# An attention batch in plain fp32, with its own order of stages on each engine, ahead of a two-layer feed-forward kernel

## The reference

```python
k_p = k.reshape(B, H, Sp, pool, D).mean(axis=3)          # B = 8, H = 8, S = 576, Sp = 72, pool = 8, D = 64
v_p = v.reshape(B, H, Sp, pool, D).mean(axis=3)
scores = scale * np.matmul(q, k_p.transpose(0, 1, 3, 2))
scores = scores - np.max(scores, axis=-1, keepdims=True)
attn = np.exp(scores)
attn = attn / (np.sum(attn, axis=-1, keepdims=True) + 1e-09)
x = np.matmul(attn, v_p)                                  # then (4608, 512)
h = x @ w_in;   x = np.maximum(0.01 * h, h) @ w_out       # w_in 512x2048, w_out 2048x512
h = x @ w_in2;  x = (h * np.clip(h + 3, 0, 6) / 6) @ w_out2
```

## Time and profile before

| | us |
|---|---|
| median of 3 runs | 1704.76 (1704.0 to 1704.78) |
| the profiled execution's own time | 1704.56 |
| its span, first to last instruction | 1702.8 |
| PE busy | 1675.4, 98% of the span |
| DVE, ACT, POOL busy | 1007.7, 627.9, 395.3 |
| start of the first tile on PE | 44.13 |
| end of the eight parts of its step 0 | 50.97 |

### The profile page before, as it was taken

One profiled execution on the slowest core, in us unless ns is written; L12 is line 12 of the kernel. 1 busy time (PEld: TensorE's weight loads), 2 busy tenths in 40 slices (PEclk: granted clock), 3 DMA queues, 4 the chain that ended last, 5 costly groups with the idle time before them and its releaser, 6 DMA issues. The chain is left out here.

```text
span 1702.8 us, 32933 instructions
## 1 busy us (share of the span) xinstructions
PE 1675.4 (98%) x10460; PEld 1489.4 (87%) x10460; DVE 1007.7 (59%) x1807; ACT 627.9 (37%) x1329; POOL 395.3 (23%) x427
## 2 busy tenths in 40 slices
PE   7999999999999999999999999999999999999999
PEld 6777888888888888888999888988989898989898
DVE  6767777676676867765455555444545454444444
ACT  4544433333333433333323333333333333333333
POOL 6226551021120212112432112121111212121200
PEclk8999999999999999999999999999999999999999
DMA  6745778768686786858787757666756675757562
GB/s 197 244 154 195 260 253 247 234 202 278 197 260 222 227 261 204 273 179 280 234 271 245 251 174 227 175 222 176 223 180 222 174 226 174 227 173 227 173 202 75
DMA packets 215810, 366.83 MB, mean 215 GB/s; under 512 B 22464, under 2 KB 47040, under 8 KB 215744
## 3 DMA queue, kind: packets, MB, share of 16 engines
q1 hardware_dynamic: 215744, 366.04, 68.1%
HBM read 308.28 MB, written 57.67 MB: 215 GB/s over the span
## 5 line engine op out<-in xcount | busy, mean ns | idle before, releaser
L1431 PE MATMUL ps_h<-xs_hi,ring 128*128 128x256 f32 x3808 | 814.8, 283 | 10.6 <-ACT p L1056 4.9
L1431 PEld LDWEIGHTS ps_h<-xs_hi,ring 128*128 128x128 f32 x3808 | 642.8, 189 | 56.4 <-issue 15.9
L1431 PE MATMUL ps_h<-xs_lo,ring 128*128 128x256 f32 x1904 | 534.3, 281 | 0.0
L1431 PEld LDWEIGHTS ps_h<-xs_lo,ring 128*128 128x128 f32 x1904 | 358.1, 188 | 25.7
L939 ACT ACTIVATE g_hi<-gate 128x512 fp32r<-128x512 f32 x288 | 181.9, 632 | 397.7 <-DVE gate L1137 212.7
L1384 PE MATMUL ps_y<-g_hi,wout_hi 128*128 128x512 f32 x576 | 225.7, 392 | 0.4 <-DVE y_stage L1192 0.4
L1386 PE MATMUL ps_y<-g_hi,wout_lo 128*128 128x512 f32 x576 | 225.4, 391 | 0.0
L1385 PE MATMUL ps_y<-g_lo,wout_hi 128*128 128x512 f32 x576 | 225.2, 391 | 0.0
L1196 DVE TENSOR_TENSOR u<-ps_h,p 128x256 f32<-128x256 f32 x272 | 114.3, 420 | 186.8 <-PE ps_h L1431 152.1
L1385 PE MATMUL ps_y<-wout_lo,g_hi 128*128 128x512 f32 x576 | 224.2, 389 | 0.0
L1386 PE MATMUL ps_y<-wout_hi,g_lo 128*128 128x512 f32 x576 | 224.2, 389 | 0.0
(11 more groups left out here) (115 smaller groups left out, 1994.2 us busy)
## 6 DMA issues: line engine op xcount, KB each, us to landing
ring<-w_in_split SPq DMA_DIRECT2D x920, 256.0 KB, 2.8
w_in_split<-ring SPq DMA_DIRECT2D x56, 256.0 KB, 3.5
w_in_split<-stage SPq DMA_DIRECT2D x56, 256.0 KB, 3.6
k_raw<-in_kT SPq DMA_DIRECT2D x32, 288.0 KB, 3.8
q_raw<-in_qT SPq DMA_DIRECT2D x32, 288.0 KB, 5.3
v_raw<-in_v SPq DMA_DIRECT2D x32, 288.0 KB
x0T<-x_stage SPq DMA_DIRECT2D x32, 288.0 KB, 3.8
x1T<-y_stage SPq DMA_DIRECT2D x36, 256.0 KB, 5.0
```

The lines of the kernel that those rows point to most:

```text
L1431: mm = pe.matmul(banks[BANK_OF[r]], a, b[:, r, c, :], start=r in OPENS and c == 0 and n == 0, stop=c == 1 and n == 2, skip_group_check=True)
```

## The change

- The first batch's product with the values is one plain fp32 matmul for each head (`pT_f`, `v_f`) in the place of three fp32r matmuls. DVE's `pT_lo` and POOL's `v_sum` and `v_lo` of that batch are gone.
- The keys of units 2 and 3 are summed by DVE in one instruction each, not by POOL in three.
- `FIRST_STAGES` is replaced by three lists, one for each engine. DVE takes the scores of the next unit ahead of normalizing the one before. ACT's roundings 3 to 7 stand at the end. PE has six of the eight parts of step 0 of the first tile (`upper`, `lower`) behind and between the last stages of unit 3, and so no longer as one block.
- The turned half 1 of unit 3 uses unit 0's buffers (`half_buffers`).
- `keep_warm` stands at other places, with other counts, and writes to whichever bank is idle. Ahead of the first scores there are 8 such matmuls, not 13.

```diff
-FIRST_STAGES = [("sum_k", 0), ("sum_k", 1), ("place_k", 0), ("place_k", 1), ("scores", 0),
...
-                ("round", 7), ("turn_p1", 3), ("split_x", 2), ("pv1", 3), ("split_x", 3)]
+FIRST_DVE = [("sum_k", 0), ("sum_k", 1), ("scores", 0), ("scores", 1), ("sum_k", 2),
+             ("normalize", 0), ("divide", 0), ("scores", 2), ("sum_k", 3), ("normalize", 1),
+             ("divide", 1), ("scores", 3), ("normalize", 2), ("divide", 2), ("normalize", 3),
+             ("divide", 3), ("split_x", 0), ("split_x", 1), ("split_x", 2), ("split_x", 3)]
+FIRST_ACT = [("place_k", 0), ("place_k", 1), ("exp", 0), ("exp", 1), ("place_k", 2),
+             ("turn_p0", 0), ("exp", 2), ("pv0", 0), ("place_k", 3), ("round", 0),
+             ("turn_p1", 0), ("turn_p0", 1), ("pv1", 0), ("exp", 3), ("round", 1), ("pv0", 1),
+             ("turn_p1", 1), ("turn_p0", 2), ("split_x", 0), ("round", 2), ("pv1", 1),
+             ("pv0", 2), ("turn_p1", 2), ("turn_p0", 3), ("split_x", 1), ("pv1", 2),
+             ("turn_p1", 3), ("split_x", 2), ("pv0", 3), ("round", 3), ("pv1", 3),
+             ("split_x", 3), ("round", 4), ("round", 5), ("round", 6), ("round", 7)]
+FIRST_PE = [("scores", 0), ("scores", 1), ("scores", 2), ("turn_p0", 0), ("pv0", 0),
+            ("scores", 3), ("turn_p1", 0), ("pv1", 0), ("turn_p0", 1), ("pv0", 1),
+            ("turn_p1", 1), ("turn_p0", 2), ("pv1", 1), ("pv0", 2), ("turn_p1", 2),
+            ("turn_p0", 3), ("pv1", 2), ("turn_p1", 3), ("upper", 0), ("pv0", 3), ("upper", 1),
+            ("pv1", 3), ("upper", 2), ("lower", 0), ("lower", 1), ("lower", 2), ("upper", 3),
+            ("lower", 3)]
+
 WARM_UP = 8
-WARM_STAGES = {("place_k", 0): 0, ("place_k", 1): 3, ("scores", 0): 5, ("place_k", 2): 4,
-               ("turn_p0", 0): 8, ("pv0", 0): 5}
+WARM_STAGES = {("scores", 1): 4, ("scores", 2): 11, ("pv0", 0): 3, ("scores", 3): 5,
+               ("turn_p1", 0): 1, ("pv1", 0): 3, ("pv0", 1): 3, ("turn_p1", 1): 2,
+               ("pv0", 2): 2, ("turn_p1", 2): 2, ("pv1", 2): 1}
...
+        def half_buffers(b, c, half):
+
+            return units[0] if first(b) and c == PAIRS - 1 and half == 1 else buffers(b, c)
...
                 for hd in range(2):
-                    nc.gpsimd.tensor_tensor(u.v_hi[:, hd, hd * D:(hd + 1) * D],
+                    nc.gpsimd.tensor_tensor(u.v_f[:, hd, hd * D:(hd + 1) * D],
                                             raw_v[:, hd, :, 0], raw_v[:, hd, :, 1], ALU.add
-                                            ).then_inc(v_hi_ready, 1)
-                nc.gpsimd.tensor_tensor(u.v_sum[:], raw_v[:, :, :, 0], raw_v[:, :, :, 1],
-                                        ALU.add).then_inc(v_summed, 1)
-                pool.wait_ge(v_summed, c + 1)
-                v_lo(0, c)
+                                            ).then_inc(v_ready, 1)
+                pool.wait_ge(v_ready, 2 * c + 2)
+                pool.sem_inc(v_summed, 1)
...
-                    nc.scalar.activation(u.pT_hi[:, :, 0:n_q], u.ps[0:KEYS, :, 0:n_q], ACT.Copy
+                    to = at.pT_f if first(b) else at.pT_hi
+                    nc.scalar.activation(to[:, :, 0:n_q], at.ps[0:KEYS, :, 0:n_q], ACT.Copy
                                          ).then_inc(pT_hi_ready, 1)
...
+                    if first(b):
+                        pe.wait_ge(pT_hi_ready, half + 2 * n + 1)
+                        for hd in range(2):
+                            mm = pe.matmul(at.ps[:, half, 0:n_q], u.v_f[:, hd, :],
+                                           at.pT_f[:, hd, 0:n_q], start=hd == 0,
+                                           stop=hd == 1)
...
             def first_step(i):
...
+                if i == 0:
+
+                    for m in range(HF):
+                        place(m)
+                    return
                 first_part(i, 1, 0)
...
+            for name, c in FIRST_PE:
+                if name in ("upper", "lower"):
+                    first_part(0, int(name == "upper"), c)
+                else:
...
+                    keep_warm(WARM_STAGES.get((name, c), 0), idle)
                     stage(name, 0, c)
             for i in range(HF):
                 first_step(i)
```

More of the change, by code:

```diff
@@ L374, in wait_k_sum @@
         def wait_k_sum(eng, b, c):
-            if first(b) and c < 2:
+            if first(b):
                 eng.wait_ge(first_k_summed, c + 1)
@@ L790, in _ @@
             for u in units:
-                pool.memset(u.v_hi[:].bitcast(F32), 0.0).then_inc(v_zeroed, 1)
-                pool.memset(u.v_lo[:].bitcast(F32), 0.0).then_inc(v_zeroed, 1)
-            pool.wait_ge(v_zeroed, 2 * PAIRS)
-            pool.sem_inc(k_summed, 2)
-            sum_k(2, 0)
-            sum_v(0, 2)
-            sum_k(3, 4)
-            sum_v(1, 6)
-            sum_v(2, 8)
-            sum_v(3, 10)
+                pool.memset(u.v_f[:], 0.0).then_inc(v_zeroed, 1)
+            pool.memset(units[0].v_hi[:].bitcast(F32), 0.0).then_inc(v_zeroed, 1)
+            pool.memset(units[0].v_lo[:].bitcast(F32), 0.0).then_inc(v_zeroed, 1)
+            pool.wait_ge(v_zeroed, PAIRS + 2)
+            pool.sem_inc(k_summed, PAIRS)
+            pool.sem_inc(v_hi_ready, 2 * PAIRS)
+            pool.sem_inc(pT_ready, 2 * PAIRS)
+            for c in range(PAIRS):
+                sum_v(c, 2 * c)
             blocks_lo(0)
@@ L1474, in stage @@
                     half = int(name[-1])
+                    at = half_buffers(b, c, half)
                     pe.wait_ge(prob_ready, 2 * n + half + 1)
+                    if at is not u:
+                        pe.wait_ge(x0_copied, 2)
                     for hd in ((0, 1), (1, 0))[half]:
-                        if half == 1 and hd == 0:
+                        if half == 1 and hd == 0 and at is u:
                             pe.wait_ge(x0_copied, 2 * n + 1)
@@ L1488, in stage @@
                     half = int(name[-1])
-                    pe.wait_ge(pT_ready, 2 * n + half + 1)
+                    at = half_buffers(b, c, half)
+                    n_q = PART_QUERIES[half]
                     if half == 0:
                         pe.wait_ge(v_ready, 2 * n + 2)
-                    for hd in range(2):
-                        n_q = PART_QUERIES[half]
-                        mm = product(u.ps[:, half, 0:n_q], (u.v_hi[:, hd, :], u.v_lo[:, hd, :]),
-                                     (u.pT_hi[:, hd, 0:n_q], u.pT_lo[:, hd, 0:n_q]),
-                                     hd == 0, hd == 1)
+                    if first(b):
+                        pe.wait_ge(pT_hi_ready, half + 2 * n + 1)
[4 more added lines that the diff above has]
+                    else:
+                        pe.wait_ge(pT_ready, 2 * n + half + 1)
+                        for hd in range(2):
+                            mm = product(u.ps[:, half, 0:n_q],
+                                         (u.v_hi[:, hd, :], u.v_lo[:, hd, :]),
+                                         (u.pT_hi[:, hd, 0:n_q], u.pT_lo[:, hd, 0:n_q]),
+                                         hd == 0, hd == 1)
                     mm.then_inc(pv_done, 1)
@@ L1574, in _ @@
             pe.wait_ge(zeroed, 2)
-            keep_warm(WARM_UP)
-            pe.wait_ge(v_zeroed, 2 * PAIRS)
+            keep_warm(WARM_UP, ps_y[:, DC - 1])
+            pe.wait_ge(v_zeroed, PAIRS + 2)
             pe.wait_ge(kT_zeroed, PAIRS)
-            for i, (name, c) in enumerate(FIRST_STAGES):
-                if name in ("scores", "turn_p0", "pv0", "turn_p1", "pv1"):
-                    if i < FIRST_STAGES.index(("place_k", PAIRS - 1)):
-                        keep_warm(WARM_STAGES.get((name, c), 2))
+            idle = ps_y[:, DC - 1]
+            for name, c in FIRST_PE:
+                if name in ("upper", "lower"):
+                    first_part(0, int(name == "upper"), c)
+                else:
+                    if (name, c) == ("turn_p1", 0):
+                        pe.wait_ge(shifted, 4)
+                        idle = ps_h[:, 0]
+                    if (name, c) == ("turn_p0", 1):
+                        idle = ps_att[:, 0]
+                    keep_warm(WARM_STAGES.get((name, c), 0), idle)
                     stage(name, 0, c)
```

41 lines of the change are left out of this document (13 added, 28 removed).

## The result

| | before | changed |
|---|---|---|
| median of 10 runs each, us | 1705.18 (1704.0 to 1706.82) | 1699.78 (1696.4 to 1701.69) |
| profiled execution, us | 1704.56 | 1698.74 |
| its span, us | 1702.8 | 1696.9 |
| first `second` on PE, us | 55.04 | 47.74 |

The ratio of the changed kernel to the one before is 0.9967, with a 95% interval of 0.9957 to 0.9976. The change makes the kernel faster, by 5.4 us between the medians and 5.9 us between the profiled spans. The prediction was 1696.8 with a range of 1693.5 to 1701.5. Four of the 31 runs of the kernel before that stand beside e4 to e7 had a mean clock of 0.56 to 0.81 and took 1909 to 2751 us; they are left out of every comparison.

The account below looks back on a forecast made before the run. PE is busy 98% of the span, so gains must come from the first 55 us, where it waits for DVE and its clock falls. 10.7 - 2.8 = 7.8 off 1704.56 gives 1696.8; 8-in-10 range 1693.5 to 1701.5.

Parts of the forecast that it names:

- The head: PE's start: shorter warm-up brings first scores to 5.3 from 6.69, but the first turn only to 13.8 from 13.95.
- The price of a plain product: First batch's product with the values on PE: 0.86 ns per plain fp32 column and record, `pv0` 1.31, `pv1` 0.66.
- From 19.4 PE sets the pace: First batch from 19.4: PE's work 20.4 plus waits 0.5 ends step 0's parts at 40.3, 10.7 earlier.
- the split of 5.5 and 5.2: Gain of 10.7 by the end of step 0's parts: 5.5 from the clock, 5.2 from DVE's path and filled waits.
- What is late next: SP's queue: late block 3 delays batch 1's values to 37.5, landing 41.0; PE waits 2.8, first `second` at 47.2.
- the waits that follow are the same: Behind the first `second`: ACT, DVE and PE stand to each other as before, only 7.8 earlier.
- rival B: Clock falls: at PE's wait at 44, loss 6.8, 1703.6, chance 0.05; as early as 18, 1717, chance 0.06 for slower.
- rival C: Later in the tile: what PE wins in the first batch is waited for again; 1702 to 1706, chance 0.06.
- The sum: Whole kernel: 10.7 - 2.8 = 7.8 off the profiled 1704.56 gives 1696.8.
- Rival A: SP's queue decides: values, or raw weights and keys behind them, land late; 1700.6 to 1702.7, chance 0.13.

Follow-up runs that it names:

- e4: Changed kernel without the identity matmuls between the stages of the first batch; median 1709.50 us, ratio 1.0018 to the kernel before.
- e7: Changed kernel with 13 instead of 8 warm-up matmuls ahead of the first scores; median 1700.21 us, ratio 0.9963 to the kernel before.
- e0: The changed kernel run again with no edit; median 1700.58 us, ratio 0.9965 to the kernel before.
- e6: Changed kernel with its new order kept but the values' products split into fp32r parts again; median 1708.32 us, ratio 1.0014 to the kernel before.
- e2: Changed kernel with DVE's `v_sum` of batch 1's first values, and ACT's rounding of them, moved later; median 1697.81 us, ratio 0.9957 to the kernel before.
- e1: Changed kernel with ACT's rounding of block 3 moved to right behind block 2; median 1697.24 us, ratio 0.9953 to the kernel before.
- e10: Same edit as e1, run again for a second profile; median 1697.10 us, ratio 0.9950 to the kernel before.
- e3: Changed kernel with 15 identity matmuls filling PE's wait ahead of the first `second`; median 1698.66 us, ratio 0.9958 to the kernel before.
- e8: Changed kernel with the edits of e1 and e2 and five identity matmuls ahead of the first `second`; median 1697.97 us, ratio 0.9954 to the kernel before.
- e9: Changed kernel with e1's edit and five identity matmuls ahead of the first `second`; median 1698.11 us, ratio 0.9960 to the kernel before.

## Why the prediction was right, and where it was off

**The head.** First scores at 5.05 (5.3 predicted), first turn at 12.72 (13.8). The 1.1 won there varies: in e0's profile the clock rose later and the parts slipped by as much. In e7 five more warm-ups made no difference in time.

**The price of a plain product.** `pv0` is issued in 1.37 (15.92-14.55) against 1.31 predicted. That is two matmuls of 384 columns, 1.78 ns for a column, 3.9 times the 0.46 of an fp32r product. The Trainium skill, "FP8 and Floating Point Precision", section "TensorE Precision Notes", says that true fp32 takes four passes, and this agrees. The six fp32r products of `pv0` in the kernel before took 1.14 (16.69 to 17.83), so on PE the plain product is the dearer one; what it saves is DVE's `pT_lo` and the wait for it.

**From 19.4 PE sets the pace.** Right. Predicted were DVE's last division over by 28.7 at the latest, no gap over 0.8, 0.5 of waits and the parts issued by 40.3. Measured: 25.97, no wait over 0.3, 0.3 of waits and 39.76. Two errors partly cancel in the last number: PE had issued unit 3's scores by 18.48 and not by 19.4, and from there it took 21.3 and not 20.9. The 11.2 won by this point (10.7 predicted) is made of the two things that the prediction named. The clock is the cleaner of them: e4 takes it away again. The path through DVE comes back in e6, but with a low stretch of 6.8 beside it, so the split of 5.5 and 5.2 between the two is not shown.

**What is late next.** Right in every link: block 3 rounded on ACT at 34.80 (35.4 predicted), POOL done with it and A12 free to go at 36.0 (36.5), v issued at 36.92 (37.5), in DVE's hands at 41.24 (41.0). PE's wait was 3.8 against 2.8: it was ready at 43.95 instead of 44.4, and the chain to `wout_lo` ended 0.4 later. So the first `second` stood at 47.74 against 47.2, a gain of 7.3 instead of 7.8. The landing in 3.5 was the short end of 3.4 to 9.5, chosen because little else would be on its way; it took 4.3, and 3.8 to 4.4 in the five other profiles of this kind. The DMA share from 34 to 38 was 0.30, so the reason held, and it was not luck. e2 shows that the wait is 1.2 once `v_sum` is out of the chain.

**The step that was off** is the sentence that behind this point the engines stand as before, "only 7.8 earlier, and the waits that follow are the same". The tail is 1649.2 against 1647.8, so 1.4 was given back. The first part of it is the small version of rival B. It was set aside because a wait of 2.42 had left the clock alone; here a wait of 2.7 to 5.0 came with a low stretch of 3.4 to 6.8 in all six profiles with such a wait unfilled (changed, e0, e1, e6, e7, e10), and so did the 1.92 of e4, while none came with the 1.2 and 2.1 of e2's profile or with the filled waits. By the mean clocks it came in 15 of the 17 runs of this kernel. The prediction gave it a chance of 0.05, a length of 13.7 and a price of 6.8; it costs 0.5 for 3.4 low us and 1.7 for 6.8, by the table at e3. So the prediction took this loss to be far too rare, and far too dear. The other 0.9 of the 1.4 comes in the long loop at full clock: the changed kernel's `g_hi` stand 7.3 earlier than before at 375 us, 6.9 at 700 and 5.8 at 1500. There PE's waits by line grow only from 4.9 to 5.5 for ACT's `p` and from 0.4 to 0.9 for DVE's `h`. That looks like rival C in small, but no run shows the cause.

**The sum.** 1696.8 + 0.5 (wait) + 1.4 (tail) gives the profiled 1698.7. The remaining 1.0 to the median is the spread of the runs: the one that was profiled is the second fastest of its ten. Rival A did not come: v landed within 4.3 of its issue. e1's profile shows that the same load can take 11.2 when it is issued into a full DMA stretch.

**What stays open.** Why the tail grows by 1 to 2 us in the long loop when the front is early (from the sixth `g_hi` on e8 takes 1.9 more than e3, e9 1.1, at a clock of 1.00 in all three) was not settled. Nor was why runs at a clock of 1.000 still differ by 3.4 us (e9). From 60 to 330 us the waits of PE for other engines in e3, e8 and e9 agree to 0.1. One profile for each kernel doesn't separate this from a drift between runs.

## What to carry to other kernels

When an engine is rid of a wait, walk the queues to what it meets next, and price the clock behind that wait as well: behind a wait of PE of 3.9 us the low clock took 1.7 more by the next checkpoint, and identity products in the wait kept the clock up in all five runs and took 1.9 off the median. Price a low clock by what it delays and not by half its length, since later waits take up part of it. Test an order of stages with the operations that it was made for and with the old ones: here the same order with the old products was slower than the old order. Check what stands on a shared in-order queue behind a step that is moved late: here a rounding that looked free on ACT set the time of a load three places on.
